# Where the zero rows of a sorted token buffer are written, and which operand of the gate product is stationary, in an attention and mixture-of-experts kernel

## What is computed

```
x   = attention(q, k, v)            # 2 batches, 8 heads, 768 positions, head size 64; local window of 16 plus 24 block summaries
                                    # rearranged to x[1536, 512]
logits = x @ w_gate + modality_bias[modality_id]          # w_gate[512, 8]: 8 experts
e_idx  = argmax(logits); gate_w = softmax(logits)[e_idx]
for e in range(8): out[e_idx == e] = gate_w * (relu(x @ w1[e]) @ w2[e])    # 512 -> 1024 -> 512
y = relu(out @ w_in) ** 2 @ w_out                          # 512 -> 2048 -> 512
```

## Time and profile before

| | us |
|---|---|
| median of 3 runs | 522.28 |
| lowest, highest | 520.22, 523.31 |
| profiled execution, its own time | 521.77 |
| its span, first to last instruction | 520.1 |
| PE busy in the span | 508.1 |
| DVE busy in the span | 225.4 |
| ACT busy in the span | 188.0 |

### The profile page before, as it was taken

The page is one execution under the profiler, slowest core; times in us unless marked ns, Lnnn a source line. Parts: engine busy times, 40 slices in busy tenths (PEclk is TensorE's granted clock), DMA queues, the critical chain, the costliest instruction groups (busy, mean ns, idle before and its releaser), DMA issues.

```text
span 520.1 us, 9415 instructions
## 1 busy us (share of the span) xinstructions
PE 508.1 (98%) x3115; PEld 410.0 (79%) x3117; DVE 225.4 (43%) x440; ACT 188.0 (36%) x355; POOL 87.1 (17%) x110
## 2 busy tenths in 40 slices
PE   8889999999999999999999999999999999999995
PEld 3678788888888888888788888888888888888884
DVE  4787686974323554237632422342242233222221
ACT  1876665243524544225522212331221233122121
POOL 4434335027600223100000000300000020000002
PEclk9999999999999999999999999999999999999999
DMA  8999666384661655521200000400000020000002
GB/s 285 336 290 340 235 220 228 99 285 104 189 216 41 219 204 202 202 82 40 83 1 1 0 1 0 161 0 0 0 0 0 0 81 0 0 0 0 0 0 81
DMA packets 19018, 54.92 MB, mean 106 GB/s; under 512 B 2848, under 2 KB 3120, under 8 KB 18480
## 3 DMA queue, kind: packets, MB, share of 16 engines
q1 hardware_dynamic: 11200, 27.47, 16.6%
q0 software_dynamic: 5200, 23.62, 12.6%
q10 hardware_dynamic: 2592, 3.49, 1.8%
HBM read 42.51 MB, written 12.07 MB: 105 GB/s over the span
## 4 chain that ended last, share of the span: by engine, by line
PE 95%; DVE 3%; issue 1%; ACT 1%; POOL 0%; POOLq 0%; DVEq 0%; ACTq 0%
PE psum L1653 9%; PE psum L1654 9%; PE psum L1652 9%; PE psum L1668 8%; PE psum L1669 8%; PE psum L1670 8%; PE psum L1536 5%; PE psum L1559 5%; PE psum L1538 5%; PE psum L1560 5%; PE psum L1561 5%; PE psum L1537 5%; PE psum L1396 2%; PE psum L1569 2%; PE psum L1371 2%; PE psum L1456 2%
## 5 line engine op out<-in xcount | busy, mean ns | idle before, releaser
L1326 DVE TENSOR_TENSOR sq<-r_sb 128x512 f32<-128x512 f32 x48 | 33.2, 692 | 141.4 <-ACT r_sb L734 137.4
L734 ACT ACTIVATE r_sb<-psum 128x512 f32<-128x512 f32 x48 | 28.7, 597 | 143.7 <-PE psum L1654 143.7
L1668 PE MATMUL psum<-W,s_hi 128*128 128x512 f32 x192 | 75.9, 395 | 0.1
L1653 PE MATMUL psum<-z_lo,W 128*128 128x512 f32 x192 | 75.8, 395 | 0.0
L1654 PE MATMUL psum<-z_hi,W 128*128 128x512 f32 x192 | 75.8, 395 | 0.0
L1652 PE MATMUL psum<-z_hi,W 128*128 128x512 f32 x192 | 75.8, 395 | 0.0
L1669 PE MATMUL psum<-W,s_hi 128*128 128x512 f32 x192 | 75.5, 393 | 0.0
L1670 PE MATMUL psum<-W,s_lo 128*128 128x512 f32 x192 | 75.4, 393 | 0.0
L893 POOL DMA_INDIRECT out<-o_sb,sorted_m x12 | 11.6, 969 | 293.5 <-DVE o_sb L1342 291.6
L1328 DVE TENSOR_TENSOR s_lo<-sq,s_hi 128x512 fp32r<-128x512 f32 x48 | 33.2, 692 | 33.5 <-ACT s_hi L736 33.5
L736 ACT ACTIVATE s_hi<-sq 128x512 fp32r<-128x512 f32 x48 | 30.3, 632 | 41.8 <-DVE sq L1326 41.8
(11 more groups left out here) (205 smaller groups left out, 729.5 us busy)
## 6 DMA issues: line engine op xcount, KB each, us to landing
raw<-in_w POOLq DMA_DIRECT2D x4, 2048.0 KB, 9.1
raw<-in_w_io POOLq DMA_DIRECT2D x4, 2048.0 KB, 8.2
v_in<-in_v SPq DMA_DIRECT2D x12, 390.0 KB, 12.7
raw<-in_w SPq DMA_DIRECT2D x8, 512.0 KB, 4.3
kT<-in_kT SPq DMA_DIRECT2D x8, 400.0 KB, 7.9
q_in<-in_q SPq DMA_DIRECT2D x12, 256.0 KB, 8.8
X<-in_vT SPq DMA_DIRECT2D x4, 768.0 KB, 11.7
x_in<-xs_d SPq DMA_DIRECT2D x12, 256.0 KB, 2.8
```

The costliest lines, as they stand in the source:

```text
L1326: dve.tensor_tensor(sq[:, :], r_sb[:, :], r_sb[:, :], ALU.mult).then_inc(sem["sqs"], 1)
L1653: pe.matmul(bank[f % 2][:, :], wh, z_lo[:, k, :], start=False, stop=False)
L1668: pe.matmul(bank[2 + j][:, :], s_hi[f % SBUFS][:, tok], wh, start=(f == 0), stop=False)
```

## The change

Two things are changed.

*Gate product.* For the blocks 0 to 6 (`TILED` = 7) the weights are stationary and the block moves. `w_gate` is padded from 8 to 32 columns for each slice k (`GCOLS`). The new `gate_parts(i-3)` stands on PE in the steps 3 to 9, between `values` and `turn`: four products, one for each slice, each into its own group of 32 columns of the array, and so into 32 partitions of a [128, 128] area `lp_bank` behind the results of `values` in PSUM. DVE's new `gate_copy(i-3)` copies this area to `part_l`; it stands behind `row_max` and before `norm`, and waits for `sem["lp"]`. In the next step `gate_sums` takes the place of `gate_logits` at the head of `scores`: one product with `part_l` stationary and 8 moving columns of a constant `gate_sum` of zeros and ones, which adds the four parts. It waits for `sem["lpc"]`, DVE's copy. ACT's `xT_copy` waits for `lp` instead of `lg`. The blocks 7 to 11 keep `gate_logits`. One small DMA on ACT's queue loads `gate_sum` behind `w_gate`.

*Zero rows.* The four DMAs of L474 go away. POOL waits for the one of L471 behind the scatters of the groups 0 and 1. `EROWS` becomes 1664. Once the counts are known, DVE computes with three operations a row for each expert: right behind its tokens when it has fewer than 128, and behind the 1536th row of its region otherwise. SP reads these eight rows and issues eight DMAs of 128 zero rows, between the load of tile 2 and that of tile 3, and waits until all have landed before it loads tile 3.

```diff
-EROWS = N
+EROWS = N + P
+GCOLS = P // KD
+TILED = NB - 5
+    sums = np.zeros((P, E), np.float32)
+    for j in range(KD):
+        sums[j * GCOLS:j * GCOLS + E] = np.eye(E)
-    w_gate = sb("w", "w_gate", [P, KD, E], F32)
+    w_gate = sb("w", "w_gate", [P, KD, GCOLS], F32)
+    lp_bank = bO[0][:, PAIRS * (D + 1):PAIRS * (D + 1) + P]
@@ SP, its loop and behind it
-                if ZFIRST <= i < ZFIRST + E // ZSTEP:
-                    some = slice((i - ZFIRST) * ZSTEP, (i - ZFIRST + 1) * ZSTEP)
-                    sp.dma_start(xs_d[P:, :].rearrange("(e r) d -> r e d", e=E)[0:P, some], wide(zero[:, :], 1, ZSTEP)
-                                 ).then_inc(sem["zfill"], 16)
             sp.dma_start(x_in[0][:, :], xs_d[bass.ds(row, P), :]).then_inc(s_xs[0], 16)
+            sp.wait_ge(sem["pads"], 1)
+            for t in range(2):
+                sp.wait_ge(s_x0[t], 16)
+            for n in range(E):
+                pad = sp.value_load(table[0:1, T_PAD + n:T_PAD + n + 1], min_val=P, max_val=E * EROWS)
+                sp.dma_start(xs_d[bass.ds(pad, P), :], zero[:, :]).then_inc(sem["zpad"], 16)
             sp.wait_ge(sem["rows"], 1)
+            sp.wait_ge(sem["zpad"], E * 16)
@@ ACT
+            act.dma_start(gate_sum[:, :], a["cf"][:, CF["gate_sum"][0]:CF["gate_sum"][1]]).then_inc(sem["w_gate"], 16)
             def xT_copy(i):
                 act.wait_ge(sem["xt"], i + 1)
-                if i:
+                if 0 < i <= TILED:
+                    act.wait_ge(sem["lp"], i)
+                elif i:
                     act.wait_ge(sem["lg"], i)
@@ POOL
-            pool.wait_ge(sem["zfill"], (1 + E // ZSTEP) * 16)
             scatter(0)
             scatter(1)
+            pool.wait_ge(sem["zfill"], 16)
@@ DVE
+            def gate_copy(i):
+                dve.wait_ge(sem["lp"], i + 1)
+                if i:
+                    dve.wait_ge(sem["lg"], i)
+                dve.tensor_copy(part_l[:, :], lp_bank).then_inc(sem["lpc"], 1)
@@ DVE, step i, behind row_max(i + 1), before norm(i - 2)
+                if 3 <= i < 3 + TILED:
+                    gate_copy(i - 3)
@@ DVE, before lsub (L1140)
+            r(dve.tensor_scalar(pad_f[:, 0, :], cnt[:, :], float(P), float(N), ALU.is_ge, ALU.mult))
+            r(dve.tensor_tensor(pad_f[:, 1, :], pad_f[:, 0, :], cnt[:, :], ALU.max))
+            dve.tensor_tensor(table[:, T_PAD:T_PAD + E], pad_f[:, 1, :], cfv("base"), ALU.add).then_inc(sem["pads"], 1)
@@ PE
                 if i >= 5:
-                    gate_logits(i - 5)
+                    gate_sums(i - 5)
+            def gate_parts(i):
+                pe.wait_ge(sem["xtc"], i + 1)
+                if i:
+                    pe.wait_ge(sem["lpc"], i)
+                for k in range(KD):
+                    ins = pe.matmul(lp_bank[k * GCOLS:(k + 1) * GCOLS, :], w_gate[:, k, :], xT[:, k, :], start=True, stop=True)
+                ins.then_inc(sem["lp"], 1)
+            def gate_sums(i):
+                pe.wait_ge(sem["lpc"], i + 1)
+                pe.matmul(lg_bank(i)[:, LG0:LG0 + E], part_l[:, :], gate_sum[:, :], start=True, stop=True
+                          ).then_inc(sem["lg"], 1)
@@ PE, step i, behind values(i - 2)
+                if 3 <= i < 3 + TILED:
+                    gate_parts(i - 3)
```

More of the change, by code:

```diff
@@ L66 @@
 T_X0 = T_E0 + 1
-T_ALL = T_X0 + SPEC
+T_PAD = T_X0 + SPEC
+T_ALL = T_PAD + E
 AHEAD = 1
+GCOLS = P // KD
+TILED = NB - 5
 VPITCH = 9 * P
@@ L79 @@
 EARLY = 1
-ZFIRST, ZSTEP = NBS - 1, 2
+ZFIRST = NBS - 1
 FRAC = 16
@@ L93, in _columns @@
     return at
-NCF = _columns(CF, ident=P, thr=LEAST, tile=TILES + 1, tile_row=TILES + 1, base=E, run=E, rank=E, spec=SPEC, seen=SPEC - 1, token=NB)
+NCF = _columns(CF, ident=P, gate_sum=E, thr=LEAST, tile=TILES + 1, tile_row=TILES + 1, base=E, run=E, rank=E, spec=SPEC, seen=SPEC - 1, token=NB)
 NCB = _columns(CB, ident=P, below=P, ones=P, mask=3 * KEYS, base=E, frac=E)
@@ L110, in constants @@
     put(f, CF, "ident", eye)
+    sums = np.zeros((P, E), np.float32)
+    for j in range(KD):
+        sums[j * GCOLS:j * GCOLS + E] = np.eye(E)
+    put(f, CF, "gate_sum", sums)
     put(f, CF, "thr", P * np.arange(LEAST)[None])
@@ L191, in build @@
     xT = sb("w", "xT", [P, KD, P], F32)
-    w_gate = sb("w", "w_gate", [P, KD, E], F32)
+    w_gate = sb("w", "w_gate", [P, KD, GCOLS], F32)
+    gate_sum = sb("w", "gate_sum", [P, E], F32)
+    part_l = sb("w", "part_l", [P, P], F32)
     warm = sb("w", "warm", [P, 512], BF16)
@@ L223, in build @@
     skip = sb("t", "skip", [P, E], F32)
+    pad_f = sb("t", "pad_f", [P, 2, E], F32)
     tiles = sb("t", "tiles", [P, E], F32)
@@ L328, in build @@
     names = """const const_r ident w_gate mbias cleared zero ones bias_ok logit rk
-        ksum kw sc mx ex tr0 tr1 pt0 pt1 pv norm xt xtc lg rank oneh rowd vtsum sums vm vsum
+        ksum kw sc mx lp lpc ex tr0 tr1 pt0 pt1 pv norm xt xtc lg rank oneh rowd vtsum sums vm vsum
         meta metas sorted rows placed slots rout oh tab n_run e0 x0 warm early lsub scat_b scat_c scat_d x2
-        raw0 raw1 zfill scat_a x_t x_h x_l l1 relu ht hh hl l2 y sh sla slbv slbp
+        raw0 raw1 zfill pads zpad scat_a x_t x_h x_l l1 relu ht hh hl l2 y sh sla slbv slbp
         counts both ylast wo_h wo_v zin scale zt zh zl m1 r sqs s_h s_l mo o_a o_v out ofree den_ok""".split()
@@ L1410, in gate_logits @@
                 for k in range(KD):
-                    ins = pe.matmul(lg_bank(i)[:, LG0:LG0 + E], xT[:, k, :], w_gate[:, k, :], start=(k == 0),
+                    ins = pe.matmul(lg_bank(i)[:, LG0:LG0 + E], xT[:, k, :], w_gate[:, k, 0:E], start=(k == 0),
                                     stop=(k == KD - 1))
                 ins.then_inc(sem["lg"], 1)
+            def gate_parts(i):
[9 more added lines that the diff above has]
+                          ).then_inc(sem["lg"], 1)
             def ranks(g):
@@ L1462, in _ @@
             pe.wait_ge(sem["ident"], 16)
-            pe.wait_ge(sem["w_gate"], 16)
+            pe.wait_ge(sem["w_gate"], 32)
             for i in range(NB):
@@ L1703 @@
     vt = v.reshape(B, PAIRS, 2, S, D).transpose(0, 2, 4, 1, 3).reshape(B, P, PAIRS, S)
-    gate = moe_w_gate.reshape(KD, P, E).transpose(1, 0, 2)
+    gate = np.pad(moe_w_gate.reshape(KD, P, E).transpose(1, 0, 2), ((0, 0), (0, 0), (0, GCOLS - E)))
     ids = moe_modality_id.view(np.int32).reshape(NB, P, 2).transpose(1, 0, 2)
```

## The result

The changed kernel takes 535.6 us (median of 4 runs, 530.32 to 537.30), the kernel before, measured beside it, 521.26 (4 runs). The ratio is 1.023, interval 1.0181 to 1.0279: 2.3% slower where I had forecast no change. Medians are of all runs; ratios and their intervals are of the runs in the faster of the two states in which a kernel can be found, so that a ratio can differ a little from the quotient of the medians. The profiled execution took 534.69 us with a span of 532.2, against 521.77 and 520.1 before.

The account below looks back on a forecast made before the run. PE's own work or stops were taken to bound the kernel (508.1 of 520.1 us busy). Loop -0.33, removed fill -0.53 and DVE operations +0.48 gave -0.4: 521.9 us against 522.28, range 519.8 to 525.0.

Parts of the forecast that it names:

- step (b): SP's eight row reads and DMAs before tile 3: 9.3 us, landed at 107.1; covered with 5.9 us to spare.
- (d): The 2 MB of zero rows collide with the first 2 MB weight load, needed only from the eighth tile, 160 us.
- tile 3 comes late: Rival: if SP's read and issue exceeds 1.9 us, PE stands before tile 3's transposes; at 2.5 us each, 526.9; chance 0.03.
- The gap at 37.1: PE's 1.06 us gap without releaser in the attention loop; half taken as gone with the zero fill, -0.53 us.
- Gate logits: Gate product on PE in the attention loop: 0.59 us replaces 0.81, gaining 0.22 per step, 1.5 at most.
- the first rival: Column groups do not overlap in the gate parts: 0.65 us more per step, 525.2 to 526.4; chance 0.09.
- the loop as a whole: Attention loop's sum of PE gains, DVE's later norm and the first tile's way: -0.33 us.
- step (a): Three small DVE operations computing the zero rows, ahead of the next tiles' x_lo and h_lo: +0.48 us on PE, uncovered.

Follow-up runs that it names:

- after: The changed kernel itself, with gate parts and zero rows behind the counts, against the kernel before: 535.6 us, ratio 1.023.
- late3: Kernel before with tiles 64 bytes further on, plus four awaited 64-byte writes by SP ahead of tile 3's request: 523.83 us.
- fill_one: Kernel before with one 256 KB zero write in place of the four wide ones: 521.06 us, ratio 0.9981.
- shift_only: Kernel before with a table eight unused columns longer, so tiles behind it move 32 bytes: 523.73 us, ratio 1.0024.
- shift_128: Kernel before with 32 unused table columns, so tiles behind it move 128 bytes: 524.78 us, ratio 1.0016.
- after_even: Changed kernel with eight more unused table columns, so tiles lie 64 bytes from their place before: 523.09 us, ratio 0.9997.
- gate_only: Kernel before with only the gate product changed; zero fill and table length as before: 522.75 us, ratio 1.0021.
- const_rows: Changed kernel with the eight zero rows at constant places, so SP reads nothing from the table: 527.39 us, ratio 1.008.
- gate_64: Kernel before with only the gate product changed and sixteen unused table columns (tiles 64 bytes on): 518.43 us, ratio 0.9924.
- load3_first: Changed kernel, tiles 64 bytes on, tile 3 requested after six zero rows without waiting for landing: 519.38 us, ratio 0.9943.
- pads_only: Kernel before with only the zero rows changed; gate product as before: 531.16 us, ratio 1.0166.
- pads_even: Kernel before with only the zero rows changed, plus eight more unused table columns (tiles 64 bytes on): 526.12 us, ratio 1.0065.
- shift_64: Kernel before with sixteen unused table columns, so tiles behind it move 64 bytes: 516.38 us, ratio 0.9889.
- no_land_wait: Changed kernel with SP's wait for the zero rows' landing moved from before tile 3 to before tile 4: 529.82 us, ratio 1.0146.

## Why the prediction was wrong

**The table's zero rows, step (b).** This failed, in two places. I took the transposes at 116.68 for tile 3's. They are tile 4's. Tile 3's stand inside `layer2(1)`, between its sixth and seventh part, at 108.41 in the timeline shown above. The code says so (`layer2(1, ..., between=((6, lambda: x_transpose(3, 1, 1)),))`); I had only looked for the next transposes behind the load, and did not count them from the front. Asked for at 104.24 and 3.5 us on its way, tile 3 had 0.7 us to spare and not 5.9. By this count my own landing time of 110.8 meant a stop of 2.4 us. Second, I gave the last row 3.5 us to land, and it took 7.3 (the three last took 6.1 to 7.3, the five before them 2.0 to 2.3), because I had put the collision with the weights on the weights' side only (d) and not on the rows', for whose landing SP waits. The price of the eight issues was right: 97.24 to 105.33 is 1.16 us each.

**The price of a stop.** The rival "tile 3 comes late" had 0.03 and the right consequence from the wrong cause: it wanted reads above 1.9 us. It counted only the stop; the slow stretch behind it, 2.58 us in after and 2.4 in late3, was missing. Over the seven traces with a stop of 3.07 to 6.25 us, tile 3 to tile 4 takes 1.4 to 2.7 us longer than in a kernel of the same place without a stop.

**The table's length.** I costed the table's eight columns as work on DVE and not as a move of every tile behind them. 1.3 to 1.6 us, which no row of the kernel before could have priced.

**The gap at 37.1.** I took half of it as gone with the fill. The fill alone gives 1.0 to 1.4 us (fill_one, not told from nothing), more than the 0.53; but in six of the eight traces that also have the gate parts a gap of 2.0 to 3.3 us stands at the rank products. What I had costed as a sum of two parts is not one: 522.75 and 521.06 apart, 525.92 together. It may be most of the 2.35 us of the first stretch; it is not shown, since kernels with the attention of before reach tile 2's transposes anywhere from 95.09 (shift_only) to 98.04 (shift_128), and after_even, with a gap of at most 0.3, at 100.76. I had no rival for it.

**Gate logits.** Right in their parts. The timeline of step 5 in after:

```profile
37.15 0.16 PEld L1451 LDWEIGHTS psum<-xT,w_gate 128*32 128x32 f32 x8
37.51 0.85 PEld L1412 LDWEIGHTS psum<-ident,prob 128*120 128x120 f32 x8 [0.20 <-issue]
37.64 0.29 DVE L978 COPY part_l<-psum 128x128 f32<-128x128 f32 x1 [0.20 <-PE psum L1451]
38.33 0.30 PEld L1456 LDWEIGHTS psum<-gate_sum,part_l 128*128 128x128 f32 x2
38.47 0.21 PEld L1393 LDWEIGHTS psum<-cb 128*128 128x128 bf16 x2
40.22 0.85 PEld L1402 LDWEIGHTS psum<-k_in,q_in 64*64 64x64 f32 x32 [1.54 <-issue]
```

`gate_parts` takes 0.36 us to `turn` (0.37 predicted), the copy 0.29 (0.28), the sums 0.14 (0.22). So the four column groups do run side by side, and the first rival falls. PE gains 0.31 us a step, and at 40.25 it has nothing to do with it: it waits 1.11 us for q, a transfer that comes when it comes. That the loop as a whole gives next to nothing came out (-0.33 predicted, +0.6 to +1.1 measured in gate_only, with an interval of -0.2 to +2.3); the sign is not shown, and at the place 64 bytes on the gate parts lose 2.

**Operations on DVE, step (a).** Right: from 95.52 to 96.01 in after, 0.49 us, and from the transposes of h to the first product of tile 2 PE takes 1.21 us where it took 0.79, and the weight load in front of that product waits the 0.42 us for DVE's `x_lo`.

The median is then made of 522.3, +1.4 for the place and +3.6 for the gate parts without the wide fill, which is 527.3 (const_rows, with no late tile, took 527.39), and +8.2 for the late tile: 535.5. Only the 527.3 is a test of this sum; the 8.2 is itself the difference between after and const_rows. The sum holds for the places of before and of after. 64 bytes on, gate_64, load3_first and after_even lie at 518.4, 519.4 and 523.1, so that the late tile costs only 3.7 there, yet 9.7 without the gate parts. From tile 2's to tile 4's transposes the traces agree better: the late tile costs 7.0 us there in after (against const_rows), 7.5 in pads_only (against before), 5.6 in after_even (against load3_first) and 8.1 in pads_even (against shift_64). The rest of the difference lies outside this stretch, and I can't say where.

## What to carry to other kernels

Before a load is called covered, find its consumer by name and count, not the next one of its kind, and take the slack from there. When a wait is put in front of a load, ask which other transfer shares the DMA engines during that wait, and price a stop of PE with what the clock takes behind it: 4.7 us of stop cost 7.2 in after, 1.8 us only itself in no_land_wait. Look also at what releases the load today: in the kernel before it was DVE's table of rows, with 0.7 us to spare, and any wait put behind that word shows at once. When an edit changes the size of one tile, keep the place of the others (pad it) while measuring, or a few bytes decide over 1%.

## What the runs showed that I had not expected

The place of tiles in SBUF, moved in steps of 32 bytes with no other edit, changes the recorded length of 128x512 products from 389 to 396 ns and the kernel from 516.4 to 523.7 us or more. Two edits, neither of which can be told from nothing alone, cost 3.1 to 3.6 us together, and in most of their traces PE has a gap without a releaser. A write of 256 KB landed in 2.0 us until another engine's 2 MB load had set out, and in 6.1 to 7.3 us behind it. Behind eight writes of which seven were of 2 KB, SP still waited 5.5 us from the end of the last issue, with those 2 MB under way; behind eight of 256 KB each it was 7.8 (105.66 to 113.42).
